# Attention and two feed-forward layers on one core: ScalarE's Silu for gate times sigmoid, and another order for the next chunk's norm, the copies out of PSUM and the weight loads

## The chip, the cores and the metric

The kernel runs on one NeuronCore of a Trainium2 chip. The metric is the device time of one execution in microseconds. The engines are PE (TensorE), DVE (VectorE), ACT (ScalarE) and POOL (GpSimd); SP (SyncE) issues nearly all DMAs.

## What is computed

```python
def _attn_ref(q, k, v):                    # B, H, S, D = 4, 8, 576, 64
...
    out_d = sm_attn(q_d, k_d, v_d)         # on means over 4 positions
    out_up = np.repeat(out_d, factor, axis=2)
    mask = np.abs(pos[:, None] - pos[None, :]) < factor
...
    return (out_up + out_local).astype(np.float32)

def _moe_ref(x, w_gate, w_val, w_out, rms_g):      # 2304 x 512, d_ff 1536
    rms = np.sqrt(np.mean(x * x, axis=-1, keepdims=True) + 1e-06)
    xn = x / rms * rms_g
    g = xn @ w_gate
    silu = g * (1.0 / (1.0 + np.exp(-g)))
    val = xn @ w_val
    return (silu * val @ w_out).astype(np.float32)

def _moe2_ref(x, w_in, w_out):                     # d_ff 2048
    h = x @ w_in
    r = np.maximum(h, 0.0)
    g = r * r
    return (g @ w_out).astype(np.float32)
```

The output of the attention, laid out as 2304 tokens of 512, goes through the first layer and then the second.

## The kernel before

**Numbers.** Every large matmul works on fp32 values split in two: a high part rounded to fp32r by ACT (a copy) and a low part, the value minus the high part, from DVE or POOL. A product of two such operands is three matmul passes (L1351 and its neighbours).

**Attention** is four groups of 13 units g: nine local ones (64 queries, a band of 70 keys) and four on the means. For each unit PE makes scores, DVE takes maxima and subtracts, ACT takes the exponent, DVE sums, POOL normalises (L510), PE transposes and multiplies with V, three to four units later. The tables at the top of the file (COMBINE_AT, HIGH_AT, POOL_LOW_AT, DVE_LOW_AT, DIAG_AT and others) say at which unit g a step of what comes after is done: the preparation of weight sets 0 and 1, and the norm of the first chunk. That norm has the sum of squares, a root by Newton steps on a small tile, `diagonals()` (tmp = identity times root, L557 on POOL before), a matmul that spreads it over the partitions (`spread`, L1232), and the product with x.

**The layers.** The 2304 tokens are three chunks of 768. The first layer has 12 units per chunk (units 0 to 35, 128 hidden columns each, both for gate and value), the second 8 per chunk (units 36 to 59, 256 hidden columns each). A unit's 2x2 block product is made of 7 products (p = 0 to 6) of combined weight and x blocks, in the manner of Strassen, 6 matmuls each. They go in turn into two PSUM banks, so product p+2 waits until what product p left is read: p = 0 and 2 by an ACT copy (`first_copy`, `copy_11`), the other five by a DVE sum (`add`, L1077, writing u, vt, vt, vt and gt). The last sum, p = 6, writes the second half of gt. Between the products PE works off the projection of an earlier unit (`project`, L1381, 24 matmuls, two units behind; `project2`, L1406, 36 matmuls, one unit behind) in segments after each product, whose sizes stand in SEGS and its relatives. Unit 36 carries the projections of units 34 and 35, in the segments of SEGS_LAST.

**What follows a first-layer unit.** ACT takes the sigmoid of each half of gt (`sigmoid`, L747), DVE multiplies it with gt (`gated`, L1083) and the result with vt (`valued`, L1087), ACT makes the high part of the hidden tile hb (`hidden_high`, L755) and DVE the low part (`hidden_low`, L1091). These stand in the next unit, `gated` between the sums of products 1 and 3, `hidden_low` between those of 3 and 4.

**Preparing the next unit.** SP loads the four raw blocks of weight set u+2 (`load_w`, L411 to L417; one of them into the single tile `stage`), as soon as PE has done with the old blocks; POOL combines them (L532 to L543) and makes five low parts (L549), ACT makes the seven high parts (L662), DVE two low parts (L1017). In the first 12 units the projection's weights wo are loaded too (`load_wo`, L425), with a high part on ACT (`second_high`, L667) and a low part on DVE (`second_low`, L1118).

**Preparing the next chunk.** During the first layer of a chunk, DVE and ACT make the norm of the next: squares on ACT in its units 2 and 3; sums of squares on DVE in 3 and 4; two matmuls over them in 4 (`square_sums`); the root on a 128 x 768 tile in 11 steps (`root`, L946 to L957) in units 5 to 8, three per unit; four products with x (`normalise`, L990) in unit 9; four combinations of x (`combine_x`, L1006) in unit 10; high and low parts of x (`x_high`, L697, `x_low`, L1010) in units 11 and 0. The finished sums of a chunk leave their six PSUM banks by ACT copies into xT (`keep_y`, L771), and at the end of the second layer by copies of ACT and DVE (`keep_out`).

Each engine works in the order in which its instructions are written; semaphores carry all waits between engines. The function that makes the root's steps before:

```python
                if normed:
                    for n in ROOT_PLACE.get(j, ()):
                        root(c + 1, n)
                add(u, 4)
```

Of the kernel before, what the change touches and what calls it, by code (L numbers as in the profile page):

```python
# [70 lines left out]
SEGS_LAST = (8, 8, 8, 6, 6, 6, 6)  # L71
# [9 lines left out]
COMBINE_AT = ((17, 18, 19, 20), (27, 28, 29, 30))  # L81
HIGH_AT = ((20, 20, 21, 21, 22, 22, 23), (30, 30, 31, 31, 32, 32, 33))
POOL_LOW_AT = ((21, 22, 23, 24, 25), (32, 33, 35, 36, 37))
DVE_LOW_AT = ((24, 25), (34, 35))
# [4 lines left out]
DIAG_AT = 42  # L89
# [13 lines left out]
def fused_kernel(nc, q_d, k_d, v_d, w1_d, w2_d, rms_d, out_d):  # L103
# [9 lines left out]
    with ctx:  # L113
# [149 lines left out]
        sig_done, u_done, a_done = sem("sig_done"), sem("u_done"), sem("a_done")  # L263
# [108 lines left out]
        def _(sp):  # L372
# [71 lines left out]
            for b in range(1, NG):  # L444
# [12 lines left out]
                if b == 1:  # L457
                    sp.dma_start(gvec[:, :], rms_d).then_inc(misc_in, 16)
                    load_w(0)
                    load_w(1)  # L460

            for u in range(NUF):
                if u == 0:
# [13 lines left out]
                if u + 2 < NUF:  # L477
                    load_w(u + 2)
# [6 lines left out]
        def _(pool):  # L485
# [66 lines left out]
            def diagonals():  # L552


                pool.wait_ge(nrc, 12)
                pool.wait_ge(ss_add, 3)
                nc.gpsimd.tensor_tensor(tmp[:, :].rearrange("p (a b) -> p a b", a=TT),  # L557
                                        ident[:, None, :].broadcast_to((128, TT, 128)),
                                        rs[:, 2, 0:TT, None].broadcast_to((128, TT, 128)),
                                        ALU.mult).then_inc(dg_done, 1)  # L560

# [11 lines left out]
            for g in range(G_ALL):  # L573
# [12 lines left out]
                if g == DIAG_AT:  # L586
                    diagonals()
# [12 lines left out]
        def _(act):  # L600
# [130 lines left out]
            def copy_11(u):  # L731
                act.wait_ge(pr_done, NP * u + 3)

                if u <= NU1:
                    ready(act, u_done, u)
                else:
                    act.wait_ge(r_done, 2 * (u - NU1))
                nc.scalar.copy(gt[:, 0:HC], XY[slot0(u) % 2][:, 0:HC]).then_inc(cp_done, 1)  # L738

            def sigmoid(u, half):  # L740
# [4 lines left out]
                ready(act, u_done, u)  # L745
                h = slice(HC * half, HC * half + HC)
                nc.scalar.activation(sig[:, h], gt[:, h], ACT.Sigmoid).then_inc(sig_done, 1)  # L747
# [47 lines left out]
            for u in range(NUF):  # L795
# [13 lines left out]
                if j == 2 and first and c > 0:  # L809
                    keep_y(c - 1, 0)  # L810
                    keep_y(c - 1, 1)
                if u == NU1 + 1:
                    for n in range(6):
                        keep_y(N1 - 1, n)
                if j == 1 and c > N1:
                    for t in range(0, TT, 2):
                        keep_out(c - N1 - 1, t)
# [9 lines left out]
                if j == 2 and first and c > 0:  # L827
                    keep_y(c - 1, 2)
                    keep_y(c - 1, 3)
                if 0 < u <= NU1:  # L830
                    hidden_high(u - 1)
                if j == 2 and first and c > 0:
# [656 lines left out]
```

## Time and profile before

| | us |
|---|---|
| median of three runs | 1046.35 |
| lowest, highest run | 1043.57, 1055.59 |
| the profiled execution | 1055.75 |
| its span, first to last instruction | 1054.0 |
| busy in it: PE, DVE, ACT, POOL | 971.4, 694.6, 437.7, 599.8 |

The profile is of one execution; its span leaves out 1.75 us around it. A busy PE may still run at half clock: its clock has two levels, 1.2 and 2.4 GHz, and the profile gives the granted share of the full one. The attention stage takes about the first 190 us, the first layer runs to about 657, the second to the end. Idle time of an engine counts only where another waits for it.

### The profile page before, as it was taken

Reading aid. Unit: us, or ns where it says so; the run is one execution under the profiler, and the core shown is the slowest. Engines: PE = TensorE matmul, PEld = TensorE weight load, DVE = VectorE, ACT = ScalarE, POOL = GpSimd, SP = SyncE. Lnnn points to the kernel's source line nnn. Section 1 sums busy time; section 2 is a strip of 40 time slices with the busy share of each in tenths; the row PEclk is TensorE's granted clock in tenths of the full one; section 3 lists DMA queues with packets and bytes.
Section 4 is the critical chain, followed back from the end, with each engine's and each line's share of the span. In section 5 each row is a group of like instructions: output and inputs, shape, how many; then the busy total and the mean of one; then the engine's idle time right before and its main releaser. Section 6 shows DMA issues by size and latency. Waiting matters only on the chain.

```text
span 1054.0 us, 17656 instructions
## 1 busy us (share of the span) xinstructions
PE 971.4 (92%) x6056; PEld 867.4 (82%) x6056; DVE 694.6 (66%) x1013; ACT 437.7 (42%) x1029; POOL 599.8 (57%) x628
## 2 busy tenths in 40 slices
PE   6978988799898899888999999799999999999998
PEld 5756766698788888878889999689989989988996
DVE  6665687468878857678856658655776545764443
ACT  3554436454343554333554435524434323522321
POOL 2373548478666667676767677445554545455420
PEclk9676585899998999998999999999999999999999
DMA  9729210221110111011111222122012111021001
GB/s 238 151 102 208 48 35 1 72 89 61 60 41 21 44 50 48 26 35 41 41 41 41 60 80 61 41 81 78 23 41 68 53 41 41 21 100 41 26 15 61
DMA packets 57556, 63.93 MB, mean 61 GB/s; under 512 B 5500, under 2 KB 50428, under 8 KB 57084
## 3 DMA queue, kind: packets, MB, share of 16 engines
q1 hardware_dynamic: 55884, 61.63, 21.3%
q10 hardware_dynamic: 1584, 1.18, 0.4%
q8 instruction: 49, 0.80, 0.3%
q14 instruction: 39, 0.32, 0.1%
HBM read 58.07 MB, written 4.72 MB: 60 GB/s over the span
## 4 chain that ended last, share of the span: by engine, by line
PE 62%; DVE 11%; issue 4%; ACT 2%; POOL 0%; DMA 0%; DVEq 0%; ACTq 0%
PE bank L1351 34%; PE bank L1406 19%; PE bank L1381 10%; DVE prod L1087 1%; DVE xs L1010 1%; DVE prod L1083 1%; DVE vt L1077 1%; DVE xT L990 1%; DVE tmp L952 1%; DVE tmp L954 1%; ACT xs L697 1%; DVE wst L1017 1%; ACT hb L755 1%; ACT wst L662 0%; DVE xcomb L1006 0%
## 5 line engine op out<-in xcount | busy, mean ns | idle before, releaser
L1351 PE MATMUL bank<-xs,wst 128*128 128x384 f32 x2520 | 514.9, 344 | 34.7 <-DVE vt L1077 28.0
L1351 PEld LDWEIGHTS bank<-xs,wst 128*128 128x128 f32 x2520 | 450.6, 192 | 63.0 <-issue 42.3
L549 POOL TENSOR_TENSOR wst<-wraw,wst 128x256 fp32r<-128x256 f32 x240 | 227.3, 966 | 203.5 <-ACT wst L662 203.0
L1406 PE MATMUL bank<-wo,gs 128*128 128x512 f32 x864 | 218.4, 393 | 2.9 <-ACT xT L771 2.2
L1381 PE MATMUL bank<-hb,wo 128*128 128x512 f32 x864 | 193.6, 342 | 8.2 <-ACT xT L771 4.3
L1406 PEld LDWEIGHTS bank<-wo,gs 128*128 128x128 f32 x864 | 160.3, 188 | 31.3 <-DVE wo L1118 2.5
L1381 PEld LDWEIGHTS bank<-hb,wo 128*128 128x128 f32 x864 | 149.8, 193 | 17.8 <-issue 9.1
L1077 DVE TENSOR_TENSOR vt<-u,bank 128x384 f32<-128x384 f32 x120 | 66.1, 551 | 100.3 <-PE bank L1351 100.0
L662 ACT CAST wst<-wraw 128x256 fp32r<-128x256 f32 x360 | 123.7, 408 | 8.6 <-DMA wraw<-w_dram 5.0
L1077 DVE TENSOR_TENSOR u<-m,bank 128x384 f32<-128x384 f32 x60 | 33.2, 553 | 108.3 <-PE bank L1351 99.9
L532 POOL TENSOR_TENSOR wraw<-wraw,stage 128x256 f32<-128x256 f32 x60 | 57.5, 959 | 79.0 <-DMA wraw<-w_dram 74.0
L747 ACT ACTIVATE sig<-gt 128x384 f32<-128x384 f32 x72 | 37.9, 526 | 150.7 <-DVE gt L1077 149.6
L780 ACT CAST gs<-sig 128x768 fp32r<-128x768 f32 x24 | 20.1, 838 | 169.8 <-DVE sig L1105 169.8
L543 POOL TENSOR_TENSOR wraw<-wraw 128x256 f32<-128x256 f32 x60 | 51.9, 864 | 36.4 <-PE bank L1351 36.4
L549 POOL TENSOR_TENSOR wst<-stage,wst 128x256 fp32r<-128x256 f32 x60 | 69.2, 1153 | 0.0
L705 ACT COPY m<-bank 128x384 f32<-128x384 f32 x60 | 28.7, 478 | 97.0 <-PE bank L1351 97.0
L1077 DVE TENSOR_TENSOR vt<-vt,bank 128x384 f32<-128x384 f32 x60 | 33.1, 552 | 48.8 <-PE bank L1351 47.7
L1017 DVE TENSOR_TENSOR wst<-wraw,wst 128x256 fp32r<-128x256 f32 x120 | 61.8, 515 | 4.9 <-ACT wst L662 4.9
L536 POOL TENSOR_TENSOR wraw<-wraw 128x256 f32<-128x256 f32 x60 | 57.2, 954 | 4.5
L538 POOL TENSOR_TENSOR wraw<-wraw 128x256 f32<-128x256 f32 x60 | 57.3, 955 | 0.0
L510 POOL TENSOR_TENSOR prob<-prob,sml 128x280 f32<-128x280 f32 x36 | 27.2, 755 | 51.9 <-DVE sml L899 51.7
L738 ACT COPY gt<-bank 128x384 f32<-128x384 f32 x60 | 28.9, 482 | 59.5 <-DVE prod L1083 47.4
(103 smaller groups left out, 1133.2 us busy)
## 6 DMA issues: line engine op xcount, KB each, us to landing
wraw<-w_dram SPq DMA_DIRECT2D x180, 128.0 KB, 2.3
stage<-w_dram SPq DMA_DIRECT2D x60, 128.0 KB, 2.1
woraw<-w_dram SPq DMA_DIRECT2D x28, 256.0 KB, 2.9
vquad<-v_dram SPq DMA_DIRECT2D x16, 288.0 KB
out_dram<-xT SPq DMA_DIRECT2D x18, 256.0 KB, 3.1
kp<-k_dram SPq DMA_DIRECT2D x3, 1152.0 KB, 15.4
qs<-q_dram SPq DMA_DIRECT2D x3, 1152.0 KB, 21.6
vwin<-v_dram SPq DMA_DIRECT2D x6, 512.0 KB
```

The source lines that it names most:

```text
L532: nc.gpsimd.tensor_tensor(block[4], block[3], stage[:, :], ALU.add).then_inc(wc_done, 1)
L536: nc.gpsimd.tensor_tensor(block[1], block[4], block[0], ALU.subtract).then_inc(wc_done, 1)
L538: nc.gpsimd.tensor_tensor(block[3], block[0], block[3], ALU.subtract).then_inc(wc_done, 1)
L543: nc.gpsimd.tensor_tensor(block[6], block[2], block[1], ALU.subtract).then_inc(wc_done, 1)
L549: nc.gpsimd.tensor_tensor(b[:, 1, :], w_source(w, p), b[:, 0, :].bitcast(fp32), ALU.subtract).then_inc(wlp_done, 1)
L662: nc.scalar.copy(wst[:, s, p, 0, :], w_source(w, p)).then_inc(wh_done, 1)
L747: nc.scalar.activation(sig[:, h], gt[:, h], ACT.Sigmoid).then_inc(sig_done, 1)
L1017: nc.vector.tensor_tensor(b[:, 1, :], w_source(w, p), b[:, 0, :].bitcast(fp32), ALU.subtract).then_inc(wld_done, 1)
L1077: nc.vector.tensor_tensor(out, y, x, ALU.add).then_inc(add_done, 1)
L1351: last = mm(XY[s % 2][:, 0:HC], wst[:, u % 2, p, pw, 128 * k:128 * k + 128], xs[:, p, px, k, :], start=(p not in CONTINUES and i == 0 and ...
L1381: last = mm(out, wo[:, j, pw, 128 * m:128 * m + 128], hb[u % HRING][:, px, t0:t1], start=(j == 0 and i == 0 and (half == 0 or m % 2 == 0)) ...
L1406: last = mm(ACC[t][:, :], gs[:, v % 2, m, px, 128 * t:128 * t + 128], wo[:, 2 * j + m, pw, :], start=(j == 0 and n < 18 and i == 0), stop= ...
```

## The change

- ACT applies Silu in place of the sigmoid. `gated` multiplies that with vt directly; `valued` and the semaphore u_done are gone. `copy_11` and the first half's activation wait for a_done, the signal of that one product. Either kernel has one load of ACT's function tables ahead of the first of these activations and none behind it.
- The next chunk's sums of squares, root steps, norm products and combinations, which stood behind the sum of product 3 or 4, are spread: up to two ahead of the first sum of a unit, one behind `gated`, the fourth norm product ahead of the sum of product 5.
- The first chunk's diagonals are made by DVE at attention unit 41, not by POOL at 42.
- Weight set 1 is prepared later in attention (from unit 28 to 41), set 0 one unit later; SP issues the loads of set 1 after those of the third attention group instead of ahead of them.
- In the layers, `load_w(u + 2)` stands ahead of the wo loads and, in unit 0, ahead of the wait for the end of attention. The first wo tile is split in unit 1 instead of 0.
- ACT's copies of a finished chunk are three at the end of a unit and three at the start of the next, instead of six in the later unit; copies out of the second layer in part one unit earlier.
- SEGS_LAST is (6, 6, 6, 6, 8, 8, 8), was (8, 8, 8, 6, 6, 6, 6).

```diff
-SEGS_LAST = (8, 8, 8, 6, 6, 6, 6)
+SEGS_LAST = (6, 6, 6, 6, 8, 8, 8)
...
-POOL_LOW_AT = ((21, 22, 23, 24, 25), (32, 33, 35, 36, 37))
+POOL_LOW_AT = ((22, 23, 24, 25, 26), (36, 37, 38, 39, 40))
...
-DIAG_AT = 42
+DIAG_AT = 41
...
                 if b == 1:
                     sp.dma_start(gvec[:, :], rms_d).then_inc(misc_in, 16)
                     load_w(0)
+                if b == 2:
                     load_w(1)
 
             for u in range(NUF):
+                if u + 2 < NUF:
+                    load_w(u + 2)
                 if u == 0:
...
-                if u + 2 < NUF:
-                    load_w(u + 2)
...
                 if u <= NU1:
-                    ready(act, u_done, u)
+                    ready(act, a_done, u)
...
-                nc.scalar.activation(sig[:, h], gt[:, h], ACT.Sigmoid).then_inc(sig_done, 1)
+                nc.scalar.activation(sig[:, h], gt[:, h], ACT.Silu).then_inc(sig_done, 1)
...
                 if j == 2 and first and c > 0:
-                    keep_y(c - 1, 0)
-                    keep_y(c - 1, 1)
+                    keep_y(c - 1, 3)
+                    keep_y(c - 1, 4)
+                    keep_y(c - 1, 5)
                 if u == NU1 + 1:
-                    for n in range(6):
+                    for n in range(3, 6):
                         keep_y(N1 - 1, n)
...
+                if first and j == 1 and c > 0:
+                    for n in range(3):
+                        keep_y(c - 1, n)
+                if u == NU1:
+                    for n in range(3):
+                        keep_y(N1 - 1, n)
...
-                nc.vector.tensor_tensor(prod[:, :], sig[:, :], gt[:, :], ALU.mult).then_inc(u_done, 1)
-
-            def valued(u):
-                dve.wait_ge(u_done, u + 1)
-                nc.vector.tensor_tensor(prod[:, :], prod[:, :], vt[:, :], ALU.mult).then_inc(a_done, 1)
+                nc.vector.tensor_tensor(prod[:, :], sig[:, :], vt[:, :], ALU.mult).then_inc(a_done, 1)
...
+            def norm_work(q, j, early):
+
+                for k in SUM_SQ_PLACE.get(j, ()):
+                    if early:
+                        sum_squares(q, k)
+                steps = ROOT_PLACE.get(j, ())
+                for n in steps[0:2] if early else steps[2:]:
+                    root(q, n)
+                tiles = NORM_PLACE.get(j, ())
+                for k in tiles[0:2] if early else tiles[2:3]:
+                    normalise(q, k)
...
+                if normed:
+                    norm_work(c + 1, j, True)
                 add(u, 1)
                 if 0 < u <= NU1:
                     gated(u - 1)
-                    valued(u - 1)
+                if combined:
+                    combine_x(c + 1, 2)
+                if normed:
+                    norm_work(c + 1, j, False)
```

On DVE, in one first-layer unit of the second chunk in which the third chunk's root is made (tmp, nrm and ssq are the root's tiles, hb the hidden tile), the rows from one unit's last sum to the weight part behind the fourth sum were:

```order
L1077 TENSOR_TENSOR gt<-u,bank 128x384
L1077 TENSOR_TENSOR u<-m,bank 128x384
L1083 TENSOR_TENSOR prod<-sig,gt 128x768
L1087 TENSOR_TENSOR prod<-prod,vt 128x768
L1077 TENSOR_TENSOR vt<-u,bank 128x384
L1091 TENSOR_TENSOR hb<-prod,hb 128x768
L952 TENSOR_TENSOR tmp<-nrm 128x768
L954 SCALAR_TENSOR_TENSOR tmp<-tmp,ssq 128x768
L957 SCALAR_TENSOR_TENSOR nrm<-tmp,nrm 128x768
L1077 TENSOR_TENSOR vt<-vt,bank 128x384
L1017 TENSOR_TENSOR wst<-wraw,wst 128x256
```

On the same engine at the same place they now are:

```order
L1082 TENSOR_TENSOR gt<-u,bank 128x384
L946 TENSOR_TENSOR tmp<-nrm 128x768
L948 SCALAR_TENSOR_TENSOR tmp<-tmp,ssq 128x768
L1082 TENSOR_TENSOR u<-m,bank 128x384
L1088 TENSOR_TENSOR prod<-sig,vt 128x768
L951 SCALAR_TENSOR_TENSOR nrm<-tmp,nrm 128x768
L1082 TENSOR_TENSOR vt<-u,bank 128x384
L1092 TENSOR_TENSOR hb<-prod,hb 128x768
L1082 TENSOR_TENSOR vt<-vt,bank 128x384
L1020 TENSOR_TENSOR wst<-wraw,wst 128x256
```

The first two root steps moved ahead of the first sum (u), the third behind the gate product, and one of the two gate products is gone.

On SP, at the end of the second attention group's loads, the four loads of weight set 1 (stage and wraw) left the place ahead of the third group's K (kp) and Q (qs):

```order
 L415 DMA wraw<-w_dram 128x256
 L417 DMA wraw<-w_dram 128x256
-L411 DMA stage<-w_dram 128x256
-L413 DMA wraw<-w_dram 128x256
-L415 DMA wraw<-w_dram 128x256
-L417 DMA wraw<-w_dram 128x256
 L403 DMA kp<-k_dram 128x4x576
 L450 DMA qs<-q_dram 128x2304
```

and stand behind the third group's vquad, ahead of the fourth group's K. On the same queue they come where the third group ends:

```order
 L389 DMA vwin<-v_dram 3x256
 L396 DMA vquad<-v_dram 72x4x256 x4
+L411 DMA stage<-w_dram 128x256
+L413 DMA wraw<-w_dram 128x256
+L415 DMA wraw<-w_dram 128x256
+L417 DMA wraw<-w_dram 128x256
 L403 DMA kp<-k_dram 128x4x576
 L450 DMA qs<-q_dram 128x2304
```

So K and Q of the third group no longer stand behind loads that wait for the tile `stage`, and K and Q of the fourth do.

## Rows read from the trace of the kernel before

**Rows 1.** DVE timeline, unit ends: start us, us, engine, line, op, out<-in, xcount

```profile
232.53 0.54 DVE L1077 TENSOR_TENSOR gt<-u,bank 128x384 f32<-128x384 f32 x1
...
361.91 0.54 DVE L1077 TENSOR_TENSOR gt<-u,bank 128x384 f32<-128x384 f32 x1
...
398.79 0.56 DVE L1077 TENSOR_TENSOR gt<-u,bank 128x384 f32<-128x384 f32 x1
...
524.97 0.56 DVE L1077 TENSOR_TENSOR gt<-u,bank 128x384 f32<-128x384 f32 x1 [0.26 <-PE bank L1351]
...
561.94 0.55 DVE L1077 TENSOR_TENSOR gt<-u,bank 128x384 f32<-128x384 f32 x1 [0.64 <-PE bank L1351]
...
631.10 0.56 DVE L1077 TENSOR_TENSOR gt<-u,bank 128x384 f32<-128x384 f32 x1 [0.64 <-PE bank L1351]
...
657.00 0.54 DVE L1077 TENSOR_TENSOR gt<-u,bank 128x384 f32<-128x384 f32 x1
```

**Rows 2.** busy us by window: PE, PEld, DVE, ACT, POOL; clock; DMA share, GB/s

```profile
600.00:650.00 50.00, 50.00 (x288) 47.77 (x287) 35.59 (x49) 22.01 (x52) 36.88 (x38) 1.00 0.20 64
```

**Rows 3.** timeline of all engines, first-layer unit 8 and the next

```profile
299.09 1.50 DVE L952 TENSOR_TENSOR tmp<-nrm 128x768 f32<-128x768 f32 x1
...
303.32 0.54 DVE L1077 TENSOR_TENSOR vt<-vt,bank 128x384 f32<-128x384 f32 x1
...
304.01 1.28 PE L1351 MATMUL bank<-xs,wst 128*128 128x384 f32 x6 [2.60 <-DVE vt L1077]
...
314.39 5.71 DVE L990 SCALAR_TENSOR_TENSOR xT<-xT,gvec,nrm 128x768 f32<-128x768 f32 x4
```

**Rows 4.** DVE groups by shape, 240 to 350 us: busy us, mean ns | idle

```profile
L1087 DVE TENSOR_TENSOR prod<-prod,vt 128x768 f32<-128x768 f32 x7 | 9.2, 1319 | 0.2
...
L1091 DVE TENSOR_TENSOR hb<-prod,hb 128x768 fp32r<-128x768 f32 x8 | 8.2, 1020 | 0.6 <-ACT hb L755 0.4
L1017 DVE TENSOR_TENSOR wst<-wraw,wst 128x256 fp32r<-128x256 f32 x16 | 8.2, 510 | 0.9 <-ACT wst L662 0.9
L1083 DVE TENSOR_TENSOR prod<-sig,gt 128x768 f32<-128x768 f32 x7 | 7.7, 1097 | 0.0
L1118 DVE TENSOR_TENSOR wo<-woraw,wo 128x512 fp32r<-128x512 f32 x8 | 7.0, 874 | 0.0
```

**Rows 5.** totals of waits: who waited for whom, us in total, times, longest us

```profile
PE bank L1381 <- ACT xT L771: 4.3, 2, 2.2
...
PE bank L1381 <- DVE hb L1091: 3.9, 1, 3.9
...
PE bank L1232 <- POOL tmp L557: 3.1, 1, 3.1
...
PE bank L1406 <- ACT xT L771: 2.2, 1, 2.2
```

**Rows 6.** timeline of all engines, third attention group

```profile
70.41 0.33 SPq L411 DMA_DIRECT2D stage<-w_dram  x1
...
81.85 0.44 PE L1258 MATMUL bank<-mask,identb 64*64 64x280 bf16 x2 [9.06 <-issue]
```

**Rows 7.** timeline of all engines, end of attention and first units

```profile
196.51 0.43 SPq L411 DMA_DIRECT2D stage<-w_dram  x1
...
198.97 3.10 PE L1351 MATMUL bank<-xs,wst 128*128 128x384 f32 x12 [3.09 <-ACT m L705]
...
203.34 0.73 POOL L532 TENSOR_TENSOR wraw<-wraw,stage 128x256 f32<-128x256 f32 x1 [8.73 <-DMA wraw<-w_dram]
```

**Rows 8.** the page's groups, the sigmoid: busy us, mean ns | idle before, releaser

```profile
L747 ACT ACTIVATE sig<-gt 128x384 f32<-128x384 f32 x72 | 37.9, 526 | 150.7 <-DVE gt L1077 149.6
```

**Rows 9.** the same windows' view in the attention stage

```profile
65.00:70.00 5.00, 3.67 (x40) 2.75 (x36) 3.90 (x6) 3.87 (x13) 5.00 (x5) 0.71 0.01 2
85.00:90.00 5.00, 5.00 (x46) 3.58 (x44) 2.71 (x5) 2.53 (x8) 2.16 (x3) 0.50 1.08 209
95.00:100.00 5.00, 5.00 (x95) 3.93 (x95) 4.86 (x11) 2.28 (x6) 1.34 (x2) 1.00 1.12 184
```

More of the change, by code:

```diff
@@ L826, in _ @@
                     sigmoid(u, 0)
-                if j == 2 and first and c > 0:
-                    keep_y(c - 1, 2)
-                    keep_y(c - 1, 3)
                 if 0 < u <= NU1:
                     hidden_high(u - 1)
-                if j == 2 and first and c > 0:
-                    keep_y(c - 1, 4)
-                    keep_y(c - 1, 5)
                 if leads:
@@ L843, in _ @@
                     x_high(c + 1, 4)
+                if first and j == 1 and c > 0:
[4 more added lines that the diff above has]
+                        keep_y(N1 - 1, n)
+                if j == 0 and c > N1:
+                    keep_out(c - N1 - 1, 0)
+                    keep_out(c - N1 - 1, 2)
                 if first and c + 1 < N1 and j in (2, 3):
@@ L846, in _ @@
                     squares(c + 1, 2 * j - 3)
-                if u < J1:
+                if u == 1:
+                    second_high(0)
+                if 0 < u < J1:
                     second_high(u)
@@ L1040, in _ @@
                         first_root(n)
+                if g == DIAG_AT:
+                    diagonals()
                 for k in range(KT):
@@ L1149, in _ @@
                 if j == 1 and c > N1:
-                    for t in range(1, TT, 2):
-                        keep_out(c - N1 - 1, t)
-                if 0 < u <= J1:
+                    keep_out(c - N1 - 1, 3)
+                    keep_out(c - N1 - 1, 5)
+                if 1 < u <= J1:
                     second_low(u - 1)
@@ L1177, in _ @@
                     x_low(c, 6)
-                if normed:
-                    for n in ROOT_PLACE.get(j, ()):
-                        root(c + 1, n)
                 add(u, 4)
@@ L1185, in _ @@
                     x_low(c + 1, 1)
-                if combined:
-                    combine_x(c + 1, 2)
-                if normed:
-                    for k in NORM_PLACE.get(j, ()):
-                        normalise(c + 1, k)
-                    for k in SUM_SQ_PLACE.get(j, ()):
-                        sum_squares(c + 1, k)
+                if normed and j in NORM_PLACE:
+                    normalise(c + 1, NORM_PLACE[j][3])
                 add(u, 5)
@@ L1195, in _ @@
                     square(u, 1)
+                if j == 0 and c > N1:
+                    keep_out(c - N1 - 1, 1)
                 if prepares:
                     weights_low(w, DVE_LOW[1])
+                if u == 1:
+                    second_low(0)
                 if leads:
```

28 lines of the change are left out of this document (12 added, 16 removed).

## The prediction

> **What bounds the kernel now.** I read the time from one unit of work to the next first, because the last sum of a unit (DVE's write of the second half of gt) marks its end. The starts in [rows 1] give it: from 561.94 to 631.10 lie six first-layer units, 69.16 us or 11.53 each. PE is busy in all 50 us of the window from 600 to 650 [rows 2], so 11.53 is what the matmuls of such a unit need. Where the next chunk is prepared, units are longer: nine of them from 232.53 to 361.91 take 129.38, nine from 398.79 to 524.97 take 126.18. Against 18 x 11.53 = 207.5 that is 48.0 us too much. The two units from 631.10 to 657.00 take 25.90, 2.8 too much.
>
> Why, is in the timeline of one of them [rows 3]. Between the second and the third of DVE's five sums of a unit stand the low part of the hidden tile and three steps of the root. The steps alone run from 299.09 to 303.32, 4.23 us, and PE, which has two banks for its products and so can be only two products ahead, stands still for 2.60 until that sum has come. The four norm instructions, between the third and the fourth sum, are worse, 5.71 in one piece. So PE is the bound, but in 20 of 36 units it waits for DVE's order of work more than for its amount. By the means of [rows 4] a root unit of DVE is 5 sums x 0.55 + 1.10 + 1.32 + 1.02 + 2 x 0.51 + 0.87 + 4.23 = 12.3, a little over 11.53 too.
>
> The totals of waits [rows 5] name smaller losses of PE: 4.3 in two pieces for ACT's copies of the finished chunk (xT, L771), 3.9 for the last hidden tile (hb, L1091), 2.2 again for copies at the second layer's start, 3.1 for POOL's diagonals. Two larger ones lie in the order of SP. SP issues the second weight set from 70.41 on only (its stage tile is in use until then), and the K of the third attention group stands right behind it; PE is idle 9.06 before the matmul at 81.85 that needs it [rows 6]. After attention the third weight set is issued at 196.51, behind the wo loads; POOL waits 8.73 for it, and PE 3.09 for an ACT copy that stands behind the cast of wo [rows 7].
>
> **The change, part by part.**
> The gate: Silu gives gate times sigmoid, so of 1.10 + 1.32 on DVE one product goes, 36 times. It was hidden in units bound by PE, and counts in the units below. No row shows Silu. Its bounds from the nearest rows: the sigmoid's 526 ns [rows 8] below, and 5.71 for the longest piece of one operation here [rows 3] above. I take the sigmoid's. The Trainium skill ("ScalarE: Activation LUTs", section on the cubic evaluation) says that an activation costs the same per element whatever the function; by it Silu is 0.53 and the sum does not move. No run here shows it yet. The order has one table load in either kernel, ahead of the first of these activations, so no reload is added.
>
> The split of DVE's work, worked out for a root unit. A product and its share of the projection take PE 11.53 / 7 = 1.65 us, the product's own six matmuls about 1.1 of them. I count from the end of product 6 of the unit before; product 1 ends at 3.3. DVE has the last sum (0.55), wo's low part (0.87) and two root steps (2 x 1.4), is at 4.2 and ends the sum of product 1 at 4.8; PE needs it when product 3 starts, at 4 x 1.65 - 1.1 = 5.5. Then the gate product (1.10, to 5.9), one root step (1.4) and the second sum, at 7.9 where product 5 starts at 8.8; the hidden tile's low part, which waits for ACT until about 8.0, and the third sum at 9.6 where product 6 starts at 10.4; two weight parts of 0.51 and two sums, 11.7, 0.2 over the period of 11.53 and still ahead of the banks. The DVE total is 12.3 - 1.3 = 11.0. Nothing waits, with 0.4 to 0.9 to spare, so I leave 0.2 each for scatter. The norm unit has 1.5 more to do (5.71 for 4.23), two tiles ahead of the first sum, one behind the gate product, one ahead of the fourth sum: 0.5 to 1 lost; the units of the combinations and the x parts behind it lose as much each, since the x parts did not move. The matmuls over the squares, which must come as now, I put at 1 in one unit per chunk. That is 8 left of 48: 40 gained. What stands behind the added wait: PE's product 4 waits for ACT's copy of product 2 out of its bank, which waits for the gate product; that ends at 5.9, the copy (0.2 for the signal and 0.5, as ACT's activation of the same shape in [rows 8]) at 6.6, and PE needs it at 5 x 1.65 - 1.1 = 7.1. That is the tightest place. The units before the second layer lose one combination ahead of the fourth sum: 1.8 of 2.8 gained.
>
> SP's order. K, Q and V of the third group now go ahead of the second weight set, right after the first set, which no row holds up, so that nothing but their own space stands in their way and they are there before 81.85 - 9.06 = 72.8. The 9.1 of [rows 6] go whole. The second set goes later, behind the third group's vquad, which waits for DVE's sum of values: I put it at about 77, and POOL wants it at attention's unit 28, some 8 us after 73: a cover of 1 to 2 us. If it is gone, POOL's normalisations stand behind its wait. The third weight set is issued as its blocks come free, during unit 0, and I take it to have landed when POOL has ended its additions, at 203.34 - 8.73 = 194.6. POOL starts 8.7 earlier, but then ACT has seven casts and DVE the two low parts: 7.4 gained, PE's 3.09 among them. Bounds 3.1 and 8.7. wo's first load comes right behind it, when attention has ended; its cast is now at the end of unit 1 and the first projection in unit 2.
>
> The diagonals move from POOL's unit 42 to DVE's 41. DVE pays 1.0 to 1.5 for it, and while PE stood still there was nothing for DVE to sum either: 3.0 gained, bounds -1.5 and 3.1.
>
> ACT's copies of a chunk: three go to the end of the unit before, three to the start of this one, so the banks are free in time: 4 of 4.3. At the second layer's start three copies instead of six stand ahead of PE, but the first three wait in ACT until PE's sixth segment and push ACT later by 1: 0.8 of 2.2. The new segment table (6 first, 8 last) puts unit 35's projection behind product 4 instead of 3: counted from the end of product 1, PE comes to it one product (1.1) and some matmuls of the segments (0.7) later, and the hidden tile is ready one DVE product (1.3) sooner: 3.1 of 3.9. The second layer's copies out move within slack: 0.
>
> Sum: 40 + 1.8 + 9.1 + 7.4 + 3.0 + 4 + 0.8 + 3.1 = 69.2. The profiled execution took 1055.75 (span 1054.0), so 986.5 by its own time. It is the slowest of those measured; the median of the runs is 1046.35, 9.4 below. What differs between executions is likely waits and the clock that falls in them, partly the same that go here, so I take half of it: 982.
>
> **The rivals.**
> DVE stays the bound (A). For: 12.3 - 1.3 = 11.0 is within 5% of 11.53, and instructions over the same 768 elements take from 1.02 (mean of L1091) to 1.50 (L952), which could be what POOL does beside them; its work grows denser as units shorten. The copy chain above has 0.5 to spare. Against: the second nine units have no wo part (0.87 less). If each of the 18 units kept 1.3 more than I say, the gain is 23 less: 1005.
>
> Attention gives nothing back (B): the second weight set comes late to POOL, whose wait delays normalisations, or K of the fourth group does, and the 12 us become -3 to 3. For: each SP wait holds all loads behind it. Against: those loads are issued earlier than now, and the fourth group is no nearer to the third. 982 + 12 = 994.
>
> The clock comes back in attention (C). In 65:70 it is at 0.71, in 85:90 at 0.50 (1.2 GHz) and PE gets through 46 matmuls, in 95:100 at 1.00 and 95 matmuls [rows 9]. If the third group runs at the full clock, the 10 us of half speed after the gap are worth 5 more: 977. Against: it had fallen before the gap, while PE was still working 3.67 of 5 us. The Trainium skill ("TensorE: Matmul & The Clock Gate", on HAM oscillation) says an idle gap puts the clock back to half. By that rule the gap is the cause and C holds; by the row it is only part of it.
>
> Silu is dear (D), the case on the other side. ACT does it twice in a unit, once ahead of the first copy of the next unit. The copy of product 0 has to be out 3 x 1.65 - 1.1 = 3.8 after product 6, and 1.5 of that are the last sum, the copy and signals, so up to 2.3 per Silu costs nothing; from there every us costs each of 35 units one. From 4.3 on it eats the whole gain; at 5, 35 x 2.7 = 94 against 69: 1071. For it speaks only that no row has it.
>
> **How the numbers follow.** My forecast 0.52 (970 to 996), A 0.20, B 0.12, C 0.12, D 0.03, and 0.01 that the moves cancel. The range takes in A and C with their scatter: 964 to 1012. A measurement of this kernel can tell about 1% from no change. Faster by over 1%: 0.95; within 1%: 0.02; slower: 0.03.
>
> **What would show it.** Right: units at 11.5 to 12 between the gt sums in all of the first layer; no 9 us gap in PE at 73; Silu at 0.53; the fifth unit of a chunk and the norm unit the longest; attention some 12 us shorter, the third weight set at work some 8 us earlier; PE's waits for vt (L1077's successor) under 5 us in all. Wrong: root units above 13 with PE waiting for a DVE sum or for ACT's copy of product 2; POOL waiting for weights in attention; a Silu over 2 us; a second layer whose steady units are not as long as now.

## The result, and the profile after

| | before | changed | forecast |
|---|---|---|---|
| median, us | 1049.45 (4 runs) | 980.0 (4 runs) | 982, range 964 to 1012 |
| lowest and highest | 1043.57, 1055.59 | 975.69, 987.0 | |
| profiled execution, span | 1054.0 | 973.9 | |

The ratio is 0.9344, with a 95% interval of 0.9263 to 0.9426. Between the medians lie 69.4 us, between the two profiled spans 80.1. The unit ends on DVE, as in [rows 1], stand in the changed kernel at (start us, us, engine, line, op, out<-in):

```profile
203.37 0.55 DVE L1082 TENSOR_TENSOR gt<-u,bank 128x384 f32<-128x384 f32 x1 [0.64 <-PE bank L1365]
...
311.39 0.55 DVE L1082 TENSOR_TENSOR gt<-u,bank 128x384 f32<-128x384 f32 x1 [0.19 <-PE bank L1365]
...
345.93 0.56 DVE L1082 TENSOR_TENSOR gt<-u,bank 128x384 f32<-128x384 f32 x1 [0.20 <-PE bank L1365]
...
452.65 0.55 DVE L1082 TENSOR_TENSOR gt<-u,bank 128x384 f32<-128x384 f32 x1 [0.18 <-PE bank L1365]
...
487.19 0.55 DVE L1082 TENSOR_TENSOR gt<-u,bank 128x384 f32<-128x384 f32 x1 [0.20 <-PE bank L1365]
...
556.35 0.56 DVE L1082 TENSOR_TENSOR gt<-u,bank 128x384 f32<-128x384 f32 x1 [0.20 <-PE bank L1365]
...
582.33 0.54 DVE L1082 TENSOR_TENSOR gt<-u,bank 128x384 f32<-128x384 f32 x1
```

The first nine prepared units take 311.39 - 203.37 = 108.02 us where they took 129.38, the second nine 106.72 where they took 126.18: 40.8 less, and 7.2 above 18 x 11.53. Six plain units still take 69.16 (487.19 to 556.35). The two units up to 582.33 take 25.98 where 25.90 was before. By stretch, read at these sums (us):

| stretch | before | changed | less | forecast |
|---|---|---|---|---|
| attention and unit 0 | 193.82 | 171.56 | 22.3 | 12.1 |
| units 1, 2 | 26.90 | 20.17 | 6.7 | 7.4 |
| units 4 to 12 and 16 to 24 | 255.56 | 214.74 | 40.8 | 40 |
| units 14 and 26 (copies of a chunk) | 27.58 | 22.76 | 4.8 | 4 |
| units 34 to 36 | 44.90 | 40.65 | 4.3 | 4.9 |
| unit 37 | 17.34 | 16.23 | 1.1 | 0.8 |
| all others | 487.9 | 487.8 | 0.1 | 0 |

Not all of this is waiting. PE's 6056 matmuls keep it busy 971.4 us in the profiled execution before and 939.7 after: 31.7 of the 80.1 us are the same matmuls in less time, 48.4 less waiting. The two prepared stretches, before and then changed (us, PE, PEld, DVE, ACT, POOL; clock; DMA share, GB/s):

```profile
232.53:361.91 129.38, 113.51 (x600) 104.74 (x599) 105.37 (x130) 54.73 (x125) 90.54 (x86) 0.95 0.17 52
398.79:524.97 126.18, 112.09 (x599) 103.53 (x598) 96.51 (x120) 49.64 (x115) 85.20 (x81) 0.96 0.12 38
203.37:311.39 108.02, 106.02 (x599) 99.80 (x598) 93.29 (x121) 53.03 (x123) 86.90 (x81) 1.00 0.18 57
345.93:452.65 106.72, 105.98 (x599) 99.81 (x598) 86.06 (x112) 48.97 (x115) 83.08 (x79) 1.00 0.15 44
```

PE is busy 225.6 there before and 212.0 after, 13.6 less, and idle 27.2 less. Before, the clock fell behind several of PE's standstills; after, it stays at 1.00. In attention with unit 0, PE is busy 161.8 before at a mean clock of 0.73 and 148.5 after at 0.80, 13.2 of the 22.3 us.

DVE in one of the root units of the changed kernel, the rows from one unit's last sum on:

```profile
239.60 0.56 DVE L1082 TENSOR_TENSOR gt<-u,bank 128x384 f32<-128x384 f32 x1 [0.64 <-PE bank L1365]
240.07 0.68 DVE L1119 TENSOR_TENSOR wo<-woraw,wo 128x512 fp32r<-128x512 f32 x1
240.67 1.49 DVE L946 TENSOR_TENSOR tmp<-nrm 128x768 f32<-128x768 f32 x1
242.27 1.31 DVE L948 SCALAR_TENSOR_TENSOR tmp<-tmp,ssq 128x768 f32<-128x768 f32 x1
243.51 0.54 DVE L1082 TENSOR_TENSOR u<-m,bank 128x384 f32<-128x384 f32 x1
243.97 1.03 DVE L1088 TENSOR_TENSOR prod<-sig,vt 128x768 f32<-128x768 f32 x1
244.92 1.50 DVE L951 SCALAR_TENSOR_TENSOR nrm<-tmp,nrm 128x768 f32<-128x768 f32 x1
246.34 0.54 DVE L1082 TENSOR_TENSOR vt<-u,bank 128x384 f32<-128x384 f32 x1
```

Two root steps now stand ahead of the first sum (243.51), the third between the one gate product (L1088) and the second sum (246.34). This unit takes 11.53, and PE waits for nothing in it. Read also how the rows overlap: the sum at 243.51 has 0.54, but the next row starts 0.46 later, and most rows here overlap the next by 0.07 to 0.09 in this way. A root step behind the one that it reads does not (240.67 and 242.27). ACT's Silu, in the page's groups (busy us, mean ns | idle before):

```profile
L736 ACT ACTIVATE sig<-gt 128x384 f32<-128x384 f32 x72 | 37.9, 526 | 125.7 <-DVE gt L1082 124.5
```

It takes the 526 ns of the sigmoid in [rows 8]. Of PE's waits in [rows 5] these are left (in total, times, longest):

```profile
PE bank L1246 <- DVE tmp L966: 1.9, 1, 1.9
...
PE bank L1395 <- DVE hb L1092: 1.3, 1, 1.3
...
PE bank L1420 <- ACT xT L760: 0.8, 1, 0.8
```

The wait for the diagonals went from 3.1 to 1.9 (now for DVE's tmp), that for the hidden tile from 3.9 to 1.3, and that for the copies at the second layer's start from 2.2 to 0.8. The two pieces of 4.3 in the first layer are gone. In the third attention group, where [rows 6] had PE idle 9.06 us:

```profile
47.68 0.38 SPq L403 DMA_DIRECT2D kp<-k_dram  x1
...
73.00 0.13 PEld L1272 LDWEIGHTS bank<-mask,identb 64*64 64x64 bf16 x2
...
76.64 0.54 SPq L411 DMA_DIRECT2D stage<-w_dram  x1
...
83.98 0.96 POOL L533 TENSOR_TENSOR wraw<-wraw,stage 128x256 f32<-128x256 f32 x1 [2.60 <-DMA wraw<-w_dram]
```

K is issued at 47.68, and PE starts the group at 73.00 without a wait. The second weight set follows at 76.64, and POOL waits 2.60 for it at 83.98, with its normalisations behind that wait. The windows of [rows 9] in the changed kernel, with 75:80 added:

```profile
65.00:70.00 5.00, 3.67 (x42) 2.86 (x40) 4.06 (x7) 4.43 (x16) 5.00 (x5) 0.72 0.11 28
75.00:80.00 5.00, 5.00 (x75) 3.87 (x76) 4.71 (x11) 3.71 (x11) 2.36 (x3) 1.00 0.75 217
85.00:90.00 5.00, 4.40 (x82) 3.53 (x82) 4.83 (x13) 3.15 (x8) 4.42 (x7) 1.00 1.06 328
95.00:100.00 5.00, 3.62 (x42) 2.66 (x38) 4.79 (x6) 4.81 (x17) 4.88 (x4) 0.79 0.17 36
```

The clock falls in 65:70 as before, but is back at 1.00 in 75:80, where it had stayed at 0.50 until behind 90; it falls again at 95:100. At the end of attention, where [rows 7] had POOL wait 8.73:

```profile
167.57 4.76 POOL L521 TENSOR_TENSOR xT<-xT,outd 128x576 f32<-128x576 f32 x4 [8.57 <-ACT outd L642]
...
168.42 0.33 SPq L417 DMA_DIRECT2D wraw<-w_dram  x1
...
172.29 0.73 POOL L533 TENSOR_TENSOR wraw<-wraw,stage 128x256 f32<-128x256 f32 x1
```

The last block of the third weight set (L417) is issued at 168.42, and POOL takes the set up at 172.29, right behind its additions and with no wait.

### The profile page after: what moved, and what is told of

Same layout as the page of the kernel before. It is cut to its first block, busy times and chain, and to the rows that moved or that the text cites. A ratio compares the mean times of both kernels' runs of the same rounds, so it can differ in the third digit from the quotient of the medians.

```text
span 973.9 us, 17619 instructions
## 1 busy us (share of the span) xinstructions
PE 939.7 (96%) x6056; PEld 846.1 (87%) x6056; DVE 657.6 (68%) x978; ACT 432.9 (44%) x1029; POOL 592.6 (61%) x627
## 3 DMA queue, kind: packets, MB, share of 16 engines
q1 hardware_dynamic: 55884, 61.63, 22.3%
## 4 chain that ended last, share of the span: by engine, by line
PE 83%; DVE 7%; issue 4%; POOL 3%; ACT 2%; DMA 1%; SPq 1%; ACTq 0%; DVEq 0%; POOLq 0%
PE bank L1365 43%; PE bank L1420 20%; PE bank L1395 14%; DVE xs L1013 1%; PE bank L1283 1%; PE bank L1323 1%; PE bank L1298 1%; PE bank L1277 1%; POOL prob L511 1%; PE bank L1302 1%; ACT xs L686 1%; DMA stage<-w_dram 1%; DMA kp<-k_dram 1%; POOL xcomb L562 1%; DVE mxl L870 1%
## 5 line engine op out<-in xcount | busy, mean ns | idle before, releaser
L1365 PE MATMUL bank<-xs,wst 128*128 128x384 f32 x2520 | 503.1, 339 | 5.1 <-DVE vt L1082 2.8
L1365 PEld LDWEIGHTS bank<-xs,wst 128*128 128x128 f32 x2520 | 441.5, 188 | 29.3 <-issue 10.2
L550 POOL TENSOR_TENSOR wst<-wraw,wst 128x256 fp32r<-128x256 f32 x240 | 230.6, 979 | 141.0 <-ACT wst L651 139.5
L1395 PE MATMUL bank<-hb,wo 128*128 128x512 f32 x864 | 189.0, 336 | 1.3 <-DVE hb L1092 1.3
L1395 PEld LDWEIGHTS bank<-hb,wo 128*128 128x128 f32 x864 | 146.0, 188 | 9.9 <-issue 1.6
L533 POOL TENSOR_TENSOR wraw<-wraw,stage 128x256 f32<-128x256 f32 x60 | 51.0, 849 | 93.2 <-DMA wraw<-w_dram 93.1
L1082 DVE TENSOR_TENSOR u<-m,bank 128x384 f32<-128x384 f32 x60 | 33.1, 551 | 75.1 <-PE bank L1365 68.1
L1020 DVE TENSOR_TENSOR wst<-wraw,wst 128x256 fp32r<-128x256 f32 x120 | 70.3, 586 | 1.6 <-ACT wst L651 1.6
L550 POOL TENSOR_TENSOR wst<-stage,wst 128x256 fp32r<-128x256 f32 x60 | 65.4, 1091 | 0.0
L1082 DVE TENSOR_TENSOR vt<-vt,bank 128x384 f32<-128x384 f32 x60 | 33.1, 552 | 45.7 <-PE bank L1365 45.5
L511 POOL TENSOR_TENSOR prob<-prob,sml 128x280 f32<-128x280 f32 x36 | 27.7, 770 | 41.0 <-DVE sml L893 40.8
```

The source lines that it names most:

```text
L533: nc.gpsimd.tensor_tensor(block[4], block[3], stage[:, :], ALU.add).then_inc(wc_done, 1)
L550: nc.gpsimd.tensor_tensor(b[:, 1, :], w_source(w, p), b[:, 0, :].bitcast(fp32), ALU.subtract).then_inc(wlp_done, 1)
L1020: nc.vector.tensor_tensor(b[:, 1, :], w_source(w, p), b[:, 0, :].bitcast(fp32), ALU.subtract).then_inc(wld_done, 1)
L1082: nc.vector.tensor_tensor(out, y, x, ALU.add).then_inc(add_done, 1)
L1365: last = mm(XY[s % 2][:, 0:HC], wst[:, u % 2, p, pw, 128 * k:128 * k + 128], xs[:, p, px, k, :], start=(p not in CONTINUES and i == 0 and ...
L1395: last = mm(out, wo[:, j, pw, 128 * m:128 * m + 128], hb[u % HRING][:, px, t0:t1], start=(j == 0 and i == 0 and (half == 0 or m % 2 == 0)) ...
```

## The experiments

All run on one core. The stretches come from one profile each. The medians are of four runs, except where it says one; executions of the kernel before gave medians of 1048.7 to 1050.3 beside them.

**e1: the changed kernel again.** No edit.

> The changed kernel once more, the base of the other three. Expected 980 within 6. The first nine prepared units (unit 3's end to unit 12's end, between the gt sums) 108 us, as in the first profile. If the 80 us between the two first profiles, against 69 between the medians, come from the clock in the attention stage, this profile's attention stage (to the end of unit 0) differs from 171.6 us by some us, and no stretch behind it by more than 1.

Median 979.3, ratio 0.9345 (0.932 to 0.937). Attention 172.2, the two prepared stretches 108.4 and 107.3, nothing else off by more than 0.1. So a profile of this kernel repeats to 0.6 us in each stretch of the layers. Seven more kernels below (the changed kernel, e2, e3, e4, e8, e9, e10) have the same attention code as e1, and in these eight it took from 170.3 to 178.8 (mean 174.3). Over these eight most of the scatter is in attention, and it goes with the clock there: a mean of 0.81 in the profile with 170.3 us, 0.75 in that with 178.8. Between the first profile and e1 it is small, 0.7 in attention and 1.0 in the prepared stretches.

**e2: the norm's work in its old places, Silu kept.**

```diff
+                if normed:
+                    for n in ROOT_PLACE.get(j, ()):
+                        root(c + 1, n)
                 add(u, 4)
...
+                if combined:
+                    combine_x(c + 1, 2)
+                if normed:
+                    for k in NORM_PLACE.get(j, ()):
+                        normalise(c + 1, k)
```

> The changed kernel with the norm's steps and the third combination back in their old places on DVE; Silu stays. Theory 'order' (PE stood still because 4 to 6 us of DVE work stood in one place, between two sums): root units 13.5 to 14.5 with PE waiting 2 us for a sum in each, in all 25 to 32 us more than the changed kernel. Rival 'amount' (DVE had simply too much work in those units, and the dropped product was the cure): less than 10 us more.

Median 1012.4, 33 more; the prepared stretches 123.9 and 122.8, 31.9 more than in the first profile of the changed kernel; the units with three root steps take 14.2 to 15.7. The longest of them, DVE and PE (start us, us):

```profile
256.30 1.50 DVE L946 TENSOR_TENSOR tmp<-nrm 128x768 f32<-128x768 f32 x1
...
257.90 1.31 DVE L948 SCALAR_TENSOR_TENSOR tmp<-tmp,ssq 128x768 f32<-128x768 f32 x1
...
259.31 1.29 DVE L951 SCALAR_TENSOR_TENSOR nrm<-tmp,nrm 128x768 f32<-128x768 f32 x1
...
260.53 0.54 DVE L1082 TENSOR_TENSOR vt<-vt,bank 128x384 f32<-128x384 f32 x1
...
261.22 1.27 PE L1367 MATMUL bank<-xs,wst 128*128 128x384 f32 x6 [2.46 <-DVE vt L1082]
```

DVE had only 10.1 us of work in this unit, less than PE's 11.53, and yet PE waits 2.46 for the sum at 260.53 behind three steps in a row, as in [rows 3]. That is the theory 'order'; 'amount' is out. The unit behind it has the same wait (2.45) and takes 14.22: in the one shown the clock fell to a mean of 0.90, and PE is busy 13.20 for the same matmuls (11.77 in the other). In both stretches together PE is busy 9.9 us more than in the changed kernel and idle 22.0 more, so the lower clock comes back with the old order.

**e3: the sigmoid and both products back, the split kept.**

```diff
-                nc.scalar.activation(sig[:, h], gt[:, h], ACT.Silu).then_inc(sig_done, 1)
+                nc.scalar.activation(sig[:, h], gt[:, h], ACT.Sigmoid).then_inc(sig_done, 1)
...
+            def valued(u):
+                dve.wait_ge(u_done, u + 1)
```

> The changed kernel with the sigmoid and both products on DVE; everything else stays in its new place. Theory 'order': DVE has 1.1 to 1.3 more per unit, 12.3 of 11.53 in root units, so 0.5 to 1.5 more in each of about 18 units, 8 to 20 us in all; units without norm work stay at 11.53. Rival 'amount': 25 to 35 us more. A rival that Silu itself cost ACT something: less than 5 more.

Median 989.0, ratio 0.9436 (0.9405 to 0.9468), 9.7 more. The prepared stretches are 111.7 and 108.8, 5.8 more than in the first profile, nearly all of it in the norm unit and the three behind it. The units with three root steps stay at 11.52 to 11.66, against my 0.5 to 1.5 more. DVE in one of them:

```profile
248.53 0.94 DVE L946 TENSOR_TENSOR tmp<-nrm 128x768 f32<-128x768 f32 x1
...
250.77 0.56 DVE L1082 TENSOR_TENSOR u<-m,bank 128x384 f32<-128x384 f32 x1 [0.23 <-PE bank L1370]
251.24 1.52 DVE L1088 TENSOR_TENSOR prod<-sig,gt 128x768 f32<-128x768 f32 x1
252.79 1.38 DVE L1092 TENSOR_TENSOR prod<-prod,vt 128x768 f32<-128x768 f32 x1
254.09 1.50 DVE L951 SCALAR_TENSOR_TENSOR nrm<-tmp,nrm 128x768 f32<-128x768 f32 x1
255.51 0.54 DVE L1082 TENSOR_TENSOR vt<-u,bank 128x384 f32<-128x384 f32 x1
```

Both products and a root step stand between two sums, from 251.24 to 255.51, 4.3 us in one piece, and PE does not wait. The piece lies where two products of PE run, between the sums of products 1 and 3. Unit 36 is 17.60, 2.9 more: 1.4 in PE's wait for the hidden tile (hb), and 1.5 in PE's busy time (14.93 for 13.39), since the clock fell there to a mean of 0.90. The wait:

```profile
PE bank L1400 <- DVE hb L1096: 2.7, 1, 2.7
```

**e4: both back.**

> Both undone, loads, copies and diagonals stay new. Both theories: 38 to 44 us more than the changed kernel, the 40.8 us that the prepared units lost between the two first profiles. If it is clearly less than e2 and e3 together, the two parts buy the same time; if more, each needs the other.

Median 1020.2, 40.9 more than e1; the prepared stretches 126.2 and 125.1, 36.6 more than in the first profile. e2 and e3 make 33.1 + 9.7 = 42.8. The parts nearly add up: the split is worth about 32, Silu 8 to 10. That the stretches give back 36.6 and not the 40.8 of the first two profiles is mostly PE's busy time in them, 222.0 here and 225.6 before.

**e5: the kernel before with only the third group's loads ahead of the second weight set.**

```diff
                     load_w(0)
+                if b == 2:
                     load_w(1)
```

> The kernel before with one edit: the second weight set's loads behind those of the third attention group. Theory 'gap': the 9 us standstill of PE at 73 us goes and nothing else, 9 to 10 us less in the attention stage (unit 0's end near 184). Theory 'clock': the third group then starts at or soon comes to the full clock, and a further 4 to 8 us go between attention units 26 and 37, 13 to 18 less in all.

Median 1040.8, ratio 0.9918 (0.9888 to 0.9948), 5 to 12 us less. In the profile attention and unit 0 end at 179.7, 14.1 less than in the profile of [rows 6]. The windows 75:80 and 85:90:

```profile
75.00:80.00 5.00, 5.00 (x70) 3.75 (x70) 3.86 (x9) 3.61 (x10) 2.13 (x3) 0.95 0.85 203
85.00:90.00 5.00, 3.74 (x40) 3.01 (x41) 1.61 (x6) 1.79 (x5) 4.48 (x7) 0.57 1.05 310
```

Here too the clock is at 0.95 in 75:80 and falls to 0.57 ten us later. From unit 26 to unit 30 (DVE's first maximum of each) it takes 10.5 us, where it took 15.2.

**e6: the same edit undone in the changed kernel.** The diff is that of e5, turned round.

> The changed kernel with the same edit undone. 'gap': 9 to 10 us more, the standstill back. 'clock': 13 to 18 more, with the units 26 to 30 at 3.7 to 3.9 us each at the half clock, as before.

Median 995.2, ratio 0.9467 (0.9423 to 0.9511), 16 more than e1. In its profile, which is of the shortest of the four executions, attention takes 183.1, 11.5 more than in the first of the changed kernel. The weight set, K and the first matmuls of the group:

```profile
70.37 0.33 SPq L411 DMA_DIRECT2D stage<-w_dram  x1
...
72.26 0.38 SPq L403 DMA_DIRECT2D kp<-k_dram  x1
...
81.25 0.44 PE L1271 MATMUL bank<-mask,identb 64*64 64x280 bf16 x2 [10.15 <-issue]
```

The standstill is back, 10.15 us, behind the same load. The clock came back sooner after it than in [rows 9], so units 26 to 30 took 11.7, not the 15 that 'clock' asked for. Between the two theories: the 9 to 10 us of the standstill are in the traces, and what comes on top depends on when the clock changes: 5 in e5's profile, 1 to 2 here. By the medians the edit is worth 9.5 in the kernel before and 16 in the changed one; the longer executions of e6 have no profile.

**e7: the diagonals on POOL at unit 42.** `diagonals()` as before the change.

> The changed kernel with the diagonals made by POOL at unit 42 again. If the move gave the 3.0 us predicted, attention is 3 us longer, with PE waiting 3.1 for POOL's tmp; since PE still waits 1.6 to 1.9 for DVE's tmp in the changed kernel, I expect 1 to 1.5 more in that wait, which the medians cannot tell from nothing.

Median 981.6, ratio 0.9348 (0.9334 to 0.9362): not to be told from e1. In the trace PE waits again:

```profile
PE bank L1247 <- POOL tmp L558: 4.3, 1, 4.3
```

4.3 where it was 1.9 and 1.6, and from attention unit 41 to 44 it takes 11.1 us instead of 7.8 and 7.5. So 2.4 to 2.7 in the wait and 3.3 to 3.6 in the place, twice what I expected here, and about the 3.0 of the prediction. The two first profiles show less: 10.2 in this place before, 7.8 after. And three other kernels with the new diagonals (e4, e6, e8) take 8.5 there.

**e8: wo's loads ahead of the weight sets, and the first wo tile split in unit 0.**

```diff
-                if u + 2 < NUF:
-                    load_w(u + 2)
                 if u == 0:
...
+                if u + 2 < NUF:
+                    load_w(u + 2)
```

> The changed kernel with wo's loads ahead of the weight sets again and the first wo tile split in unit 0. Predicted for the edit: 7.4 us. Units 1 and 2 together 26 to 27.5 us (20.17 in the changed kernel), nothing else moves. Rival: only ACT's 3.1 us wait for the wo tile counted; then 23 to 24.

Median 986.0 (979.5 to 992.0). Units 1 and 2 take 25.35 instead of 20.17. SP, PE and POOL there:

```profile
177.64 0.43 SPq L411 DMA_DIRECT2D stage<-w_dram  x1
...
180.27 5.97 PE L1361 MATMUL bank<-xs,wst 128*128 128x384 f32 x24 [3.20 <-ACT m L694]
...
182.91 0.73 POOL L533 TENSOR_TENSOR wraw<-wraw,stage 128x256 f32<-128x256 f32 x1 [7.18 <-DMA wraw<-w_dram]
```

The set is issued at 177.64, PE waits 3.20 for the copy behind the cast of wo, POOL 7.18 for the set, as in [rows 7]. The edit is worth 5.2, between the two theories: more than ACT's wait alone, less than my 26 to 27.5 for the two units. 3.5 of it is PE's waiting and 1.7 its busy time, at a mean clock of 0.87 in unit 1.

**e9: the old segment table.** SEGS_LAST = (8, 8, 8, 6, 6, 6, 6); one run, 980.3.

> The changed kernel with SEGS_LAST (8, 8, 8, 6, 6, 6, 6). Predicted for this edit: 3.1 of the 3.9 us wait for the last hidden tile. Since unit 36 is 2.9 us longer with the sigmoid back (e3) though the table is new, Silu and the table may buy the same wait. If they add up: unit 36 (14.67 in the changed kernel) at 17 to 18. If Silu alone does it: at 15 or less. One profile is enough, the stretch is read in the trace.

Neither: units 36 and 37 take 16.02 and 15.87, together 1.0 more than in the changed kernel. The clock stays at 1.00 in both. The wait for hb:

```profile
PE bank L1395 <- DVE hb L1092: 2.5, 1, 2.5
```

**e10: all six copies of a chunk in one unit again.** One run, 983.65.

```diff
                 if j == 2 and first and c > 0:
-                    keep_y(c - 1, 3)
-                    keep_y(c - 1, 4)
-                    keep_y(c - 1, 5)
+                    keep_y(c - 1, 0)
+                    keep_y(c - 1, 1)
                 if u == NU1 + 1:
-                    for n in range(3, 6):
+                    for n in range(6):
```

> The changed kernel with ACT's six copies of a finished chunk back in one unit. Expected: units 14 and 26 at 13.8 instead of 11.38 (two waits of 2.1), 4.8 us in all, and unit 37 at 17.3 or more instead of 16.23; rival: the copies' place no longer matters since ACT has less to wait for, all three as in the changed kernel.

Units 14 and 26 take 13.79 and 15.33 instead of 11.38, 6.4 more where I expected 4.8, and unit 37 19.23 instead of 16.23; 9.4 in all. The old waits are back, and unit 26 as a window:

```profile
PE bank L1394 <- ACT xT L760: 4.3, 2, 2.2
...
PE bank L1419 <- ACT xT L760: 2.2, 1, 2.2
```

```profile
465.69:481.02 15.33, 13.17 (x67) 12.22 (x66) 5.46 (x9) 7.78 (x18) 9.02 (x11) 0.89 0.11 36
```

Units 14 and 26 have the same work and the same wait of 2.2. Behind it the clock stays at 1.00 in unit 14 and falls in unit 26, to a mean of 0.89, and that costs 1.5 us more. In unit 37 it falls to 0.91 behind a wait of 2.2; in the profile before it was 1.00 there behind the same wait, and the unit took 17.34.

**e11 and e12: tries at a better kernel.**

```diff
-ROOT_AT = (38, 38, 39, 39, 39, 39, 40, 40, 40, 40, 41, 41)
-DIAG_AT = 41
+ROOT_AT = (38, 38, 38, 38, 39, 39, 39, 39, 40, 40, 40, 40)
+DIAG_AT = 40
```

> A try at a better kernel: the twelve small root steps one attention unit sooner and the diagonals at unit 40. PE waits 1.6 to 1.9 for DVE's diagonals in the changed kernel; without that wait 1.5 to 2 less in attention, which the medians (979 to 980 now) can hardly tell; the wait itself is read in the profile. Rival: PE's next wait, for ACT's copy of the first half, takes its place, and nothing is gained.

Median 976.4, ratio 0.9318 (0.9293 to 0.9343), against 0.9345 (0.932 to 0.937) of e1. The wait for DVE's tmp fell to 0.3, and one of 1.9 for ACT's copy of the first half stood there (1.7 in e1 already, 0.2 in the first profile). The intervals overlap: a gain of 3 us is possible and not shown.

> As e11, and also the spread, the norm products, the combinations and the x parts of the first chunk one unit sooner. DVE is busy 4.9 of 5 us from 130 us to the end of attention, so work moved ahead of that stretch should shorten it: 2 to 5 us less than e11. Rival: the stretch ahead is bound by DVE as well, and DVE waits for ACT's copies (norm at 44 right behind the spread): no gain or 1 to 2 more.

In e12 SPREAD_AT, NORM_AT, COMBINE_X_AT, X_HIGH_AT (but for its last) and X_LOW_AT (likewise) are one less too. Median 978.1, ratio 0.9331 (0.9309 to 0.9352): no better than e11. The rival's outcome came, not shown by its reason: in e12's trace PE's waits for POOL's prob are 5.2 in all (3.5 in e11), and 3.6 more stand ahead of its L1323 with no releaser named.

## Why the prediction was right, step by step

**The bound.** That PE waited for DVE's order and not for its amount is shown by e2: the same amount of work in the old order gives back 32 of the 40.8 us, in units in which DVE has 10.1 us of work. What the prediction does not say is that up to a third of this was the clock: of the 40.8, 27.2 is PE idle less and 13.6 PE busy less. At the full clock too a unit with a standstill has PE busy 0.2 longer (11.75 for 11.53 in e4), so by an estimate some 4 of the 13.6 are not the clock. The sum holds all the same because it took the losses from the length of the units (48.0) and not from the waits; that the clock's part would go with the waits was luck, in that no step of it argues so.

**The split and the gate, 40 forecast, 40.8 measured.** The units with three root steps run at 11.53, with 0.2 left each in the forecast, 0 in the trace. What is left, 7.2, is nearly where I put it: 1.6 in each chunk for the matmuls over the squares, between the last sums of units 4 and 5, where I had 1; 0.4 in the two norm units together, where I had 1 to 2; and 3.6 in the units behind them.

**DVE's total was mis-sized.** I had 12.3 us per root unit with two products, 11.0 with one, and so gave rival A 0.20. The rows overlap by 0.08, so a sum of durations is too large: DVE is busy 10.7 to 11.0 in such units of e3, and 9.9 to 10.3 in the changed kernel. The Trainium skill ("Perfetto Trace Analysis", section "Optimizing Scalar/DVE Operations") says that a profiled DVE latency holds a part that overlaps the next instruction; the trace agrees, with 0.54 in the record and 0.46 to the next start. For the same reason e3 leaves the root units alone, where by my totals they would have become longer. A did not happen.

**Silu.** 0.526 us, as taken; rival D falls. What it bought I had not priced by itself: about 5.8 in the norm units and behind, 2.9 in unit 36 (1.5 of it the clock), 0.6 in unit 1. In plain units nothing, as said. The 1071 of rival D is counted from the median before; from the 982 the same 94 us would give 1076.

**The loads.** The K load: 9.1 forecast, the standstill gone whole. Rival C was partly there: at the full clock, units 26 to 30 took 10.0 us instead of 15.2, the 5 us that I had put on C. But in other executions the clock falls sooner in the same stretch (e3: 27.9 us from unit 26 to 36, the changed kernel 22.2). Of B the sign came and not the price: POOL does wait for the second weight set, 2.60 at 83.98, which the prediction names as a sign of being wrong, but PE's waits for POOL's prob are 2.4 in all where they were 1.6. The weight sets of the layers: 7.4 forecast, 6.7 measured, 5.2 by e8 for that edit alone. The other 1.5 is nearly all PE's busy time: 21.7 in units 1 and 2 before, where the clock was at a mean of 0.77 in unit 1, 20.4 in e8, where it was at 0.87. After, it is 18.8 at 1.00. That the clock and not another edit makes this difference is argued.

**Diagonals:** 3.0 forecast; 3.3 to 3.6 by e7's trace, 2.3 between the two first profiles, and the medians cannot tell it from nothing.

**Units 34 to 37: right in the sum, wrong in the split.** Of the wait for the last hidden tile I gave the new table 1.8 (1.1 and 0.7) and the dropped product 1.3, 3.1 of 3.9. The wait is 3.9 with neither, 2.7 with the table alone (e3), 2.5 with Silu alone (e9) and 1.3 with both: the table takes 1.2 of it and Silu 1.4, and they add up, to 2.6. What I did not have is the clock: in unit 36 it was at a mean of 0.91 before and PE busy 15.07, at 1.00 and 13.39 after, 1.7 more of the 4.3 that the unit lost. The copies I gave 0.8 in unit 37, and it lost 1.1; the 3.0 of e10 holds a fall of the clock that the profile before does not have there. So the times of e3, e9 and e10, 6.9 together, are more than the 5.4 that went. The 1.8 for units 34 and 35 was also wrong: they are as long as before, since the fourth combination still stands ahead of the last sum (1.49 us, to 569.02); what DVE is late there PE feels only in one wait of 0.67 in unit 35 (0.60 before), and unit 36 is shorter for the rest. A unit end read at a DVE sum holds DVE's lateness as well as PE's.

**The level.** By its own profile my sum gave 986.5, 10.8 above the profiled 975.69. Of that, 22.3 - 12.1 = 10.2 lies in attention. If the stretches behind attention gave in the other executions what they gave in these two profiles, 57.8, the 69.4 between the medians leave 11.6 for attention, by this estimate close to the 12.1. The two first profiles were at opposite ends of their kernels' runs: 1055.75 is the slowest of the kernel before, 975.69 the fastest of the changed one. Taking half of the distance to the median off was a guess at just this, and that it came out is luck in part: the median before was 1046.35 of three runs then and is 1049.45 of four now. That it was attention's clock in the first profile of the kernel before too is argued, since no second profile of the kernel before was taken.

## What to carry to other kernels

An in-order engine that both frees PSUM banks and does side work can stall PE at 88% load: count, for each piece of side work between two bank-freeing instructions, the time until PE needs the second one, and cut the pieces to that; here that was worth three to four times what a dropped instruction was. Price a standstill by what the unit loses and not by the wait: behind the same wait of 2.2 us the clock stayed in one unit of e10 and fell in another, which cost 1.5 us more. Look through every DMA queue for a load that waits for a buffer and stands ahead of one that could go: two such places cost 14 us. When a wait has several possible cures, measure each alone and compare the waits as well as the times: at the last hidden tile the waits added up and the times did not, because of the clock.

## What was not expected of the hardware

PE's clock is the main source of scatter. The same attention instructions took 170.3 to 178.8 us in eight profiles, at mean clocks of 0.81 to 0.75, while the layers of the changed kernel repeated to 0.6 in each stretch. In dense matmuls too the clock can fall behind a single wait of 2.2 to 3.2 us, and not behind each: units of 13.79 and 15.33 in e10. In attention PE can be busy without a gap and still be at 1.2 GHz: the window 85:90 in [rows 9] has 5.00 of 5 us busy at 0.50, and in the changed kernel the window 85:90 has 4.40 busy at 1.00.

DVE instructions of one shape and kind differ by half: the gate product L1088 over 768 elements is 1.03 in the root unit above, 1.52 in e3's, and the root step L946 0.94 there and 1.49 above. They go with what POOL does: of 132 such rows with two inputs over 768 elements between 200 and 640 us of the changed kernel, the nine with no row of POOL beside them take 0.94 to 0.96, and each of the 72 over 1.05 us has POOL at work beside it for 0.28 us or more. The Trainium skill ("SBUF — State Buffer", section "Who interferes with whom") says that a DVE instruction with two SBUF inputs contends with a GpSimd one that reads SBUF. The durations fit that; no run here took POOL away.
